# A gated recurrence, a feed-forward part and attention on one core: block products of 32 rows alone, and squares as 32 products with 64 columns of weights

## The reference

```
for t in range(S):                      # S = 768, D = 40
    y[t]  = r[t] @ state
    Sa    = state @ a[t]
    state = state * w[t] - outer(Sa, b[t]) + outer(v[t], k[t])
```

## Time and profile before

| | us |
|---|---|
| median of 3 runs | 918.59 |
| lowest, highest | 911.92, 924.1 |
| the profiled execution, time | 923.58 |
| its span, first to last instruction | 921.9 |
| TensorE busy (matmuls), weight loads | 824.6, 597.0 |
| VectorE, ScalarE, POOL busy | 559.7, 317.4, 259.5 |
| the second part, from 404.4 us: length, TensorE busy | 517.5, 491.3 |

### The profile page before, as it was taken

How to read it: one execution, slowest core, us unless ns; L and a number is a source line. 1 busy time by engine, 2 the same in 40 slices (tenths; PEclk the granted TensorE clock), 3 DMA queues, 4 the chain that set the end, 5 groups by cost and what they waited for, 6 DMA issues and landing times.

```text
span 921.9 us, 27713 instructions
## 1 busy us (share of the span) xinstructions
PE 824.6 (89%) x11872; PEld 597.0 (65%) x11872; DVE 559.7 (61%) x1235; ACT 317.4 (34%) x741; POOL 259.5 (28%) x525
## 2 busy tenths in 40 slices
PE   3428989998999988889998999988999998999988
PEld 3428889988998988864465654545644656545555
DVE  8995795878599742136528645357464277354474
ACT  4102331323133232222227542246432266322364
POOL 2087777778778877000000000000000000000000
PEclk9999895979599798899999999999999979999999
DMA  3645575657566574620100000100001000000000
GB/s 117 153 85 122 126 163 113 134 139 140 122 157 138 113 158 102 157 78 26 44 1 15 16 15 1 43 0 23 15 8 43 1 8 22 16 1 0 1 15 30
DMA packets 130922, 61.33 MB, mean 67 GB/s; under 512 B 106544, under 2 KB 119792, under 8 KB 130800
## 3 DMA queue, kind: packets, MB, share of 16 engines
q1 hardware_dynamic: 96156, 32.61, 16.3%
q10 hardware_dynamic: 34644, 26.95, 11.3%
HBM read 45.37 MB, written 14.16 MB: 65 GB/s over the span
## 4 chain that ended last, share of the span: by engine, by line
PE 75%; DVE 11%; issue 5%; ACT 5%; POOL 2%; DMA 1%; SPq 0%; ACTq 0%; DVEq 0%
PE ps_all L808 8%; PE ps_all L792 8%; PE ps_scan L105 5%; PE ps_all L852 5%; PE ps_scan L188 4%; PE ps_all L918 4%; PE ps_all L900 4%; PE ps_all L930 4%; PE ps_scan L130 3%; PE ps_scan L167 3%; PE ps_all L795 3%; PE ps_all L802 2%; PE ps_all L835 2%; PE ps_scan L122 2%; PE ps_scan L114 2%
## 5 line engine op out<-in xcount | busy, mean ns | idle before, releaser
L328 POOL TENSOR_TENSOR t_update<-solver_then_w_down 128x133 f32<-128x133 f32 (+13 forms) x251 | 118.6, 473 | 88.1 <-DMA solver_then_w_down<-l_blocks 39.1
L330 POOL TENSOR_TENSOR solver_then_w_down<-solver_then_w_down,t_update 128x133 f32<-128x133 f32 (+13 forms) x251 | 132.7, 529 | 19.7
L105 PE MATMUL ps_scan<-decayed_a_and_eye,scaled_then_x 40*128 40x104 f32 x768 | 67.6, 345 | 46.5 <-DVE decayed_a_and_eye L362 45.2
L1129 DVE TENSOR_REDUCE minus_max<-ps_all 128x1 f32<-128x128 f32 (+5 forms) x96 | 55.3, 617 | 66.8 <-PE ps_all L904 66.8
L105 PEld LDWEIGHTS ps_scan<-decayed_a_and_eye,scaled_then_x 40*128 40x128 f32 x768 | 62.8, 252 | 48.6 <-issue 47.7
L808 PE MATMUL ps_all<-gated,solver_then_w_down 128*128 128x384 f32 x256 | 91.1, 499 | 0.0
L792 PE MATMUL ps_all<-scaled_then_x,inputs_then_w_up 128*128 128x384 f32 x256 | 88.8, 490 | 1.8 <-ACT ak_l_then_ffn L970 1.8
L1028 ACT ACTIVATE probs_t<-ps_all 128x512 f32<-128x512 f32 (+3 forms) x128 | 55.1, 452 | 69.9 <-PE ps_all L918 69.3
L808 PEld LDWEIGHTS ps_all<-gated,solver_then_w_down 128*128 128x128 f32 x256 | 46.0, 189 | 44.6 <-issue 19.1
L792 PEld LDWEIGHTS ps_all<-scaled_then_x,inputs_then_w_up 128*128 128x128 f32 x256 | 47.6, 190 | 36.3 <-ACT ak_l_then_ffn L970 6.0
L232 ACT ACTIVATE x_rhs<-ps_scan 128x320 f32<-128x320 f32 x48 | 21.0, 438 | 141.3 <-PE ps_scan L122 70.5
(11 more groups left out here) (117 smaller groups left out, 1523.8 us busy)
## 6 DMA issues: line engine op xcount, KB each, us to landing
r_t_and_v_t<-in_rv ACTq DMA_DIRECT2D x48, 160.0 KB
inputs_then_w_up<-in_x ACTq DMA_DIRECT2D x46, 160.0 KB
solver_then_w_down<-l_blocks SPq DMA_DIRECT2D x22, 256.0 KB, 4.6
uv_and_ruv<-in_v ACTq DMA_DIRECT2D x48, 80.0 KB, 3.7
y_t<-y_out SPq DMA_DIRECT2D x24, 160.0 KB
out<-out_rows SPq DMA_DIRECT2D x24, 160.0 KB, 1.8
inputs_then_w_up<-in_x ACTq DMA_DIRECT2D x46, 81.4 KB
inputs_then_w_up<-in_x ACTq DMA_DIRECT2D x46, 80.0 KB
```

The lines of the kernel that those rows point to most:

```text
L105: last = nc.tensor.matmul(PS[:, o:o + ROWS], weights, AL[c % NK][rows(h), p, :], start=True, stop=True)
L328: return (lambda: eng.tensor_tensor(tmp[:, 0:cols, 0:rest], l[:, s:s + 1, s + 1:BLK].broadcast_to(shape), t[:, 0:cols, s:s + 1].broadcast_ ...
L330: lambda: eng.tensor_tensor(t[:, 0:cols, s + 1:BLK], t[:, 0:cols, s + 1:BLK], tmp[:, 0:cols, 0:rest], ALU.subtract))
L1129: nc.vector.tensor_reduce(NM[:, v:v + 1], PS[:, first_bank(v) * 512:first_bank(v) * 512 + n], AX.X, ALU.min).then_inc(m["nm"], 1)
```

## The change

Three things are changed, all in the recurrence, and one memset is added.

- The squares are 32 products in place of 16: for each p, h and j, the 64 columns of weights `BK[..., j, :]`, with the same moving 104 columns; j = 0 writes partitions 0 to 63, j = 1 partitions 64 to 127 of the same place. Order: p, then h, then j.
- First blocks: only the upper 32 rows of each half (partitions 0 to 31 and 64 to 95), with the upper 32 x 32 corner of `DT`, into the same partitions of `PY`.
- All blocks: only the lower 32 rows of each half (32 to 63 and 96 to 127), with the lower corner. The upper rows of `PY` then are those that the first blocks left; the cross does not change the upper rows of X.
- `PY` is cleared once at the start, 128 x 320, since ScalarE's copy of Y reads all of its rows.

```diff
@@ g_products
                     o = place(2 * h, p)
-                    weights = BK[c % 2][rows(h), p, :, :].rearrange("r j t -> r (j t)")
-                    last = nc.tensor.matmul(PS[:, o:o + ROWS], weights, AL[c % NK][rows(h), p, :], start=True, stop=True)
+                    for j in range(2):
+                        last = nc.tensor.matmul(PS[own(j), o:o + ROWS], BK[c % 2][rows(h), p, j, :], AL[c % NK][rows(h), p, :],
+                                                start=True, stop=True)
@@ first_blocks
-                    last = nc.tensor.matmul(PY[own(q), seg(p, D)], DT[n % 3][own(q), p, :], XS[own(q), p, :],
-                                            start=True, stop=True)
+                    a = slice(q * C, q * C + BLK)
+                    last = nc.tensor.matmul(PY[a, seg(p, D)], DT[n % 3][a, p, 0:BLK], XS[a, p, :], start=True, stop=True)
@@ all_blocks
-                    last = nc.tensor.matmul(PY[own(q), seg(p, D)], DT[n % 3][own(q), p, :], ZS[own(q), p, :],
-                                            start=True, stop=True)
+                    b = slice(q * C + BLK, (q + 1) * C)
+                    last = nc.tensor.matmul(PY[b, seg(p, D)], DT[n % 3][b, p, BLK:C], ZS[b, p, :], start=True, stop=True)
@@ vector, setup
         for b in (0, 6):
             i = nc.vector.memset(PS[BLK:C, b * 512:(b + 2) * 512], 0.0)
+        i = nc.vector.memset(PY[:, 0:P8 * D], 0.0)
```

## The result

The changed kernel takes 924.44 us, the median of 20 runs (916.41 to 932.65); the kernel before, run beside it, 919.25 us (909.93 to 927.79). The ratio is 1.0067, 95% interval 1.0039 to 1.0095: some 6 us slower, where 906 us, 13 us faster, was forecast. In all that follows, medians are of all runs of a kernel, while ratios, clocks and times at 1.2 GHz are of its fast runs, those within 1.5% of its fastest. The profiled execution took 932.65 us, the longest of the 20; what follows rests on shares and slots, and on means over many runs where sums matter.

A forecast was written before the change was run, and what follows sets the result against it. TensorE was taken as the first bound in the recurrence, with POOL and VectorE not far behind. Gross 25.2 us less 6.8 (code), 2.3 (POOL), 0.4 (clearing Y) and 2.8 (clock) gave 12.9 us, so 906 us; range 889 to 926.

The forecast's parts named there:

- The slots: TensorE's recurrence at 2.4 GHz: squares from 1.96 to 1.55 us, first blocks from 1.06 and all blocks from 0.96 to 0.70.
- the order rival: TensorE's squares: the four tiles don't overlap, so the slot is 3.10 us; 13.7 us slower, 932 us; chance 0.09.
- The drain at a change of tile shape: TensorE ahead of the first blocks: a tile shape change that was not there before costs 0.10 us per chunk.
- Code: TensorE waiting for its instructions: 0.54 us in each warm chunk (one at 2.4 GHz), 6.8 us in all.
- one new dense place: TensorE's first blocks, squares and cross: 256 instructions in 2.95 us instead of 192 in 3.72; charged 0.54 us per warm chunk.
- The rival that the code swallows it: TensorE behind the squares: each warm chunk pays 1.65 us, 20.6 in all; gain 1.9 us, 917 us; chance 0.17.
- The clock: TensorE's recurrence: one more cold chunk (nearly all at 1.2 GHz) costs 7.0 us, weighted 0.4, so 2.8 us lost.
- The clock rival: TensorE: more pauses put more chunks at 1.2 GHz; 2.2 more cancel the 15.7 us gain, 5 more give 938; chance 0.06.
- 2.3 us: POOL, solving the inverses, sets the order from about chunk 14 to 20; 2.3 us of TensorE's gain stays there.
- 25.2 won in slots: TensorE's gross gain: 10.0 us from the squares and 15.2 us from both block products.

The follow-up runs named there:

- e11: Kernel before with only the block products cut, in rows alone (weights 32 rows by 64 columns); ratio 1.0055 to the kernel before.
- e7: Changed kernel with only one 64 column half of the squares per chunk from the second chunk on, 16 products; ratio 1.0002 to the kernel before.
- e10: Changed kernel with 64 by 32 block products in place of 32 by 32; ratio 1.0006 to the kernel before.
- e12: Changed kernel with 64 by 32 block products and one 64 column half of the squares at a time; ratio 0.9862 to the kernel before.
- e1: Kernel before with only the two block products cut to 32 x 32 corners and the Y bank cleared; ratio 1.0019.
- e9: Kernel before with only the block products cut, in columns alone (weights 64 rows by 32 columns); six runs, ratio 0.9907.
- e13: The same kernel as e9 run once more, 12 runs; ratio 0.9945 to the kernel before.
- e2: Kernel before with only the squares split into 32 products with 64 columns of weights; ratio 1.0101.
- e3: Changed kernel with PAD 54 in place of 118, moving the block borders of TensorE's code; ratio 1.013.
- e5: Kernel before with small descriptors of the inverse blocks cut to an eighth on two of three transfers; ratio 0.9895.
- e6: Changed kernel with small descriptors of the inverse blocks cut to an eighth on two of three transfers; three runs, ratio 0.9886.

## Why the prediction was wrong

**The slots: right.** Squares 1.59 us against 1.55, block products 0.69 against 0.70. Wide weights, not moved columns, bound them; e11 shows it by the other side. The four tiles overlap: 64 records in 1.59 us could not be had in strict order, which would have made 3.10, so the order rival falls, and the rule behind it (the Trainium skill, "TensorE: Matmul & The Clock Gate", Part 2: matmuls stay in program order) does not describe matmuls of different row halves here. The drain at a change of tile shape was charged 0.10 us per chunk. The group ahead of the first blocks takes 0.79 us from start to start before and 0.82 in the changed kernel, so what was added there is 0.03 us; it decides nothing.

**Code: the mechanism right, the size wrong.** "I charge it 0.54 us in each warm chunk, 12.5 x 0.54 = 6.8 us" measured 15 us more of pauses in the chain of the two profiles and 20 us more of TensorE's own waits; the experiments put the 64 instructions at 6 us (changed kernel against e7, 0.65%) and 13 us (e10 against e12, 1.4%). I priced one new dense place with the mean of L122's waits. In fact they came at eleven lines, where it had been five, up to 3.35 us long, and three times in the middle of a group of squares (3.35, 0.66 and 0.34 us). Shorter slots with the old number of instructions bring the smaller part (TensorE's waits on "issue" are 15 to 24 us in e1, e9 and e13, 27.2 and 22.5 in e7 and e12, against 18.3), the 64 added ones most of it (35 to 39 us in e2, e10 and the changed kernel). The rival that the code swallows it, at 0.17, had the size of this term more nearly: its 20.6 us is next to what was measured, the forecast's 6.8 a third to a half of it. But it ended at 917 us, still a gain, and the kernel lost; the rest is the clock's.

**The clock: the step that failed.** "One more cold chunk costs 18.6 - 11.6 = 7.0 us. I give it 0.4: 2.8 us" was to cover a chance, tied to pauses. Measured are 30 us more at 1.2 GHz, 1.8 cold chunks of 16.4 us, or about 11 us. The clock rival, at 0.06, had the direction; it too tied the loss to pauses, and alone it needed 2.2 such chunks. And the tie is wrong: e1 has the pauses nearly of before and 102 us; e9 has the same pauses as e1 (8.3 and 8.6%) and 72. What the block products lost is rows of the array at work, and the clock answered to that. I had counted only what the change takes from TensorE's time, never what it takes from its load. Pauses may have a share too: e2 keeps all its cells at work and has 91 us, with 11.7% of pauses. So two terms were too small, this one by 8 us and the code's by 8 to 14. That 924.44 us lies inside the stated range, 889 to 926, is no merit: the forecast was a gain, and the interval of the ratio lies wholly above 1.

**POOL.** Its pauses were to shrink to 15 us, because chunks would come faster. They are where they were (30.1 us in the earlier trace rows):

```profile
POOL t_update L329 <- DVE solver_then_w_down L331: 31.7, 10, 10.7
```

No time was handed on to POOL, since none was won. Where time was won, POOL's pauses do shrink, to 18.5 us in e9 and 12.3 in e12, and POOL's two lines become 14.7 and 21.7% of the chain. So the mechanism holds, but 2.3 us looks small for it: e9 and e13 keep 5 to 8.5 of 15 us. No run takes POOL's share of that apart.

**The sum, by what was measured.** 25.2 won in slots, 15 lost in pauses and 11 by the clock leaves it level; the measured loss is 6 us (4 to 9). With TensorE's own waits, 20 us in place of 15, nothing is left over. But both are one profile against another, and e3's, of the changed kernel but for its borders, has 30.4 us of such waits in place of 38.7, so that fit may be chance. One wait of this pair is in neither number: X's products waited 6.6 us for their load (`PE ps_scan L115 <- DMA uv_and_ruv<-in_v`), where before it was 0.3 us.

**What stays open.** What makes a block of code come too late in one place and not in another. The Trainium skill, "Runtime: NRT & Kernel Launch", Instruction fetch mechanics, calls the cost of a block's border mostly hidden; by the earlier trace rows, e2 and e12 it isn't in a kernel whose warm chunk has 389 + 385 instructions of TensorE in 11.6 us, 67 per us. The descriptors that e5 and e6 took away are not the cause in the main. And the effect of the rows on the clock is shown as an effect on time and clock, with its mechanism not looked into. The rows that e9 adds hold zeros, and no run adds rows with other values.

## What to carry to other kernels

When a change makes small products cheaper by cutting their tile, look at three counts, not one: the columns of the weights (they set the slot), the instructions per us of TensorE (pauses for code grew with them), and the rows of the array that work (the clock fell with them here). Cut columns and keep rows: the same slot reduction with 64 x 32 in place of 32 x 32 products is faster than both kernels here, 0.9907 (0.9872 to 0.9942) and 0.9945 (0.9906 to 0.9984), and leaves nothing out. These kernels leave the squares as they were (e9, e13). Splitting a product in two to overlap its halves pays only if the added instructions are free, and where "issue" waits already stand between the groups they are not.

## What the hardware showed unexpectedly

- Rows of zeros streamed through idle parts of the array cost no time and gave some back: 102 us at 1.2 GHz without them (e1), 78 with them (e9, e13), in slots of 0.69 us both times and a kernel of the same instructions.
- A wait on a semaphore that is satisfied long since costs TensorE's queue time: with 16 products behind such waits a slot went from 1.96 to 3.80 us (at a granted clock of 0.90).
- TensorE stood for as long as 3.35 us in the middle of a group of products, and each of the 29 pauses of over 0.5 us without a releaser ended 1.2 to 1.9 us after the end of a 16 KB packet of its instruction queue.
